# Row numbers of the first expert right after its search, and more of its product in the second search

## The reference

```
logits = x @ w_gate                      # 3072 tokens, 8 experts, 384 columns
take the pairs (token, expert) from the largest logit down; a token goes to
the first expert that still has fewer than 384 tokens
out[mask_e] = max(x[mask_e] @ w1[e], 0) @ w2[e]
```

## Time and profile before

| what | us |
|---|---|
| median of 3 runs (794.68 to 795.75) | 794.81 |
| the profiled execution, its own time | 795.84 |
| its span, first to last instruction | 794.1 |
| TensorE busy in the span | 764.5 |
| VectorE busy in the span | 631.3 |
| mean granted TensorE clock | 0.984 |

### The profile page before, as it was taken

One profiled execution on the slowest core, in us unless ns is written; L12 is line 12 of the kernel. 1 busy time (PEld: TensorE's weight loads), 2 busy tenths in 40 slices (PEclk: granted clock), 3 DMA queues, 4 the chain that ended last, 5 costly groups with the idle time before them and its releaser, 6 DMA issues.

```text
span 794.1 us, 17262 instructions
## 1 busy us (share of the span) xinstructions
PE 764.5 (96%) x6864; PEld 573.2 (72%) x6864; DVE 631.3 (80%) x1081; ACT 425.1 (54%) x703; POOL 292.2 (37%) x244
## 2 busy tenths in 40 slices
PE   8899899999999999999999999977999999999994
PEld 8799678787878787878787877645566565666662
DVE  8998999989998999998999985876776776766220
ACT  2497849595968595968596879410121221222221
POOL 4335462626272627272726260011221231222311
PEclk9999999999999999999999999995999999999998
DMA  9951257373646463656464347123423424415500
GB/s 309 387 201 52 90 203 276 124 270 128 236 164 247 138 235 141 233 192 211 155 220 152 133 154 248 44 73 138 179 98 134 190 66 184 190 46 203 219 31 31
DMA packets 47792, 133.50 MB, mean 168 GB/s; under 512 B 5344, under 2 KB 19808, under 8 KB 45664
## 3 DMA queue, kind: packets, MB, share of 16 engines
q1 hardware_dynamic: 38880, 93.07, 33.4%
q0 software_dynamic: 5376, 34.61, 11.7%
q10 hardware_dynamic: 3456, 4.72, 1.7%
HBM read 97.78 MB, written 34.60 MB: 167 GB/s over the span
## 4 chain that ended last, share of the span: by engine, by line
PE 74%; DVE 10%; issue 2%; ACT 1%; another core or an unknown queue 0%; POOL 0%; ACTq 0%; DVEq 0%
PE bank L425 71%; DVE cmp L1415 2%; PE bank L749 1%; DVE g_lo L1515 1%; DVE t_sb L1118 1%; PE bank L450 1%; PE bank L511 1%; ACT t_sb L826 1%; DVE t_sb L1494 1%; DVE inv L1037 0%; DVE t_sb L1487 0%; DVE t_sb L1490 0%; DVE cum L1028 0%; DVE thr L1432 0%
## 5 line engine op out<-in xcount | busy, mean ns | idle before, releaser
L425 PE MATMUL bank<-x_hi,win_hi 128*128 128x256 f16 (+1 forms) x606 | 159.9, 267 | 0.7 <-DVE x_lo L1100 0.7
L425 PE MATMUL bank<-x_hi,win_lo 128*128 128x256 f16 (+1 forms) x606 | 159.9, 267 | 0.0
L425 PE MATMUL bank<-x_lo,win_hi 128*128 128x256 f16 (+1 forms) x606 | 159.9, 267 | 0.0
L1646 POOL TENSOR_TENSOR g_lo<-t_sb,g_hi 128x512 f16<-128x512 f32 x88 | 123.3, 1428 | 54.3 <-ACT g_hi L826 45.8
L425 PE MATMUL bank<-wout_hi,g_hi 128*128 128x392 f16 (+1 forms) x416 | 129.0, 317 | 1.6 <-DVE wout_lo L1208 1.6
L425 PE MATMUL bank<-wout_lo,g_hi 128*128 128x392 f16 (+1 forms) x416 | 128.8, 316 | 0.0
L425 PE MATMUL bank<-wout_hi,g_lo 128*128 128x392 f16 (+1 forms) x416 | 128.7, 316 | 0.0
L826 ACT ACTIVATE g_lo<-bank 128x384 f16<-128x384 f32 x64 | 31.4, 490 | 143.6 <-PE bank L425 129.1
L1629 POOL TENSOR_TENSOR dv<-v_tok,dot 128x384 f32<-128x384 f32 x24 | 29.0, 1210 | 174.4 <-DVE dot L1067 174.4
L826 ACT ACTIVATE g_hi<-t_sb 128x512 f16<-128x512 f32 x96 | 57.3, 624 | 57.8 <-PE bank L425 53.2
L1118 DVE TENSOR_TENSOR t_sb<-t_sb,h_sb 128x512 f32<-128x512 f32 x96 | 86.5, 947 | 0.5
(11 more groups left out here) (184 smaller groups left out, 1598.2 us busy)
## 6 DMA issues: line engine op xcount, KB each, us to landing
stage<-in_moe_w SPq DMA_DIRECT2D x22, 768.0 KB, 6.4
w_split<-stage SPq DMA_DIRECT2D x22, 768.0 KB, 4.5
fold_w<-in_moe_w SPq DMA_DIRECT2D x10, 768.0 KB, 9.2
w_split<-fold_w SPq DMA_DIRECT2D x10, 768.0 KB, 7.9
wt<-in_w_turned SPq DMA_DIRECT2D x24, 258.0 KB, 2.9
kt<-in_k_turned SPq DMA_DIRECT2D x24, 256.0 KB, 2.6
rt<-in_r_turned SPq DMA_DIRECT2D x24, 256.0 KB, 2.7
r_tok<-in_r SPq DMA_DIRECT2D x24, 192.0 KB, 6.0
```

The costliest lines, as they stand in the source:

```text
L425: return nc.tensor.matmul(*a, **k)
L1646: G.tensor_tensor(g_lo[:, j * GW:(j + 1) * GW], t_sb[:, j * GW:(j + 1) * GW], g_hi[:, j * GW:(j + 1) * GW], ALU.subtract).then_inc(s["glo" ...
```

## The change

The row numbers of the first expert are made at the end of the first search and no longer inside the second. On VectorE `digits`, `numbered`, `one_hot_low` and `id_blocks` stand ahead of the pick, and `token_ids` between the pick and the start of the second search; on TensorE I and J stand behind the first ranks, between 16, 6 and 16 idle products (16 of which were there before). X of the first expert moves from behind the fifth maxima of the second search to behind the third. H0 moves from B5 to B3, H1 to A4, Y0 and H2 to B4, and Y1, H3, Y2, H4 and Y3 follow in that search, so that Y1, H4, Y2 and Y3 move there from the third. The idle products of the second search remain in two steps of four. The third search holds the seven units of the first expert that are left, Y4 to Y7 and H5 to H7, in its first four steps; its units for the second expert stay as they were.

```diff
@@ placement
+        SECOND = {("B", 2): ["X"], ("B", 3): ["H0"], ("A", 4): ["H1"], ("B", 4): ["Y0", "H2"], ("B", 5): ["Y1", "H3"],
+                  ("C", 0): ["Y2", "H4", "Y3"]}
+        THIRD = {("A", 0): ["Y4"], ("B", 0): ["H5"], ("A", 1): ["I", "Y5"], ("B", 1): ["J", "H6"], ("A", 2): ["Y6"],
+                 ("B", 2): ["H7"], ("B", 3): ["Y7"], ("B", 4): ["X"], ("B", 5): ["H0", "H1"],
+                 ("C", 0): ["H2", "Y0", "H3"]}
...
-            for u in PLACES[where]:
-                p = r - 1 if u in YOUNG + ("I", "J") else r - 2
+            for u in {1: SECOND, 2: THIRD}.get(r, PLACES).get(where, []):
+                p = r - 1 if r == 1 or u in YOUNG + ("I", "J") else r - 2
@@ TensorE
-                if r == 1:
-                    idle_products(16)
...
-                    if r == 1 and t < 4:
+                    if r == 1 and t < 2:
                         idle_products(6)
...
                 ranks(r)
+                if r == 0:
+                    idle_products(16)
+                    unit(0, "I", 0)
+                    idle_products(6)
+                    unit(0, "J", 0)
+                    idle_products(16)
                 units(r, ("C", 0), unit)
@@ VectorE
-            def low_xg(p):
+            def low_xg(p, ks=range(KT)):
...
+            def first_search():
+
+                for t in range(NSTEP - 1):
+                    filled(0, t)
+                    next_step(0, t)
+                filled(0, NSTEP - 1)
+                choose(0)
+                take_slots(0)
+                digits()
+                numbered()
+                one_hot_low()
+                id_blocks(0)
+                pick_expert(slice(0, NT))
+                one_hot_expert()
+                token_ids(0)
+                leave()
+                start_search()
+
+            def second_search():
+
+                for t in range(3):
+                    filled(1, t)
+                    next_step(1, t)
+                low_xg(0, range(0, 2))
+                filled(1, 3)
+                low_xg(0, range(2, KT))
+                next_step(1, 3)
+                filled(1, 4)
+                low_h(0, 0)
+                next_step(1, 4)
+                low_h(0, 1)
+                filled(1, 5)
+                low_h(0, 2)
+                choose(1)
+                pick_expert(slice(0, NT), lambda: low_h(0, 3))
+                one_hot_expert()
+                take_slots(1)
+                leave()
+                start_search()
+                digits()
+                numbered()
+                low_h(0, 4)
+
+            first_search()
+            second_search()
+            for r in range(2, E - 1):
...
+                f = 4 if r == 2 else 3
```

More of the change, by code:

```diff
@@ L1516, in low_h @@
                                        ALU.max, ALU.subtract).then_inc(s["hlo"], 1)
-            def low_xg(p):
+            def low_xg(p, ks=range(KT)):
                 if not 0 <= p < E:
                     return
-                for k3 in range(KT):
+                for k3 in ks:
                     dve.wait_ge(s["xgThi"], KT * p + k3 + 1)
@@ L1540, in _ @@
                 link(V.tensor_scalar(grid[t][:, :], iota_t[:, :], wid[:, t:t + 1], None, ALU.mult))
-            for r in range(E - 1):
+            def first_search():
[14 more added lines that the diff above has]
+                start_search()
@@ L1543, in _ @@
+            first_search()
+            second_search()
+            for r in range(2, E - 1):
                 new, old = r - 1, r - 2
-                if r >= 1:
-                    one_hot_low()
+                f = 4 if r == 2 else 3
+                one_hot_low()
                 filled(r, 0)
-                low_h(old, 3)
+                if r > 2:
+                    low_h(old, 3)
                 next_step(r, 0)
                 filled(r, 1)
-                if r >= 1:
-                    id_blocks(r - 1)
@@ L1552, in _ @@
-                low_h(old, 4)
+                id_blocks(r - 1)
+                low_h(old, f + 1)
                 next_step(r, 1)
-                if r >= 1:
-                    token_ids(r - 1)
+                token_ids(r - 1)
                 filled(r, 2)
-                low_h(old, 5)
+                low_h(old, f + 2)
                 next_step(r, 2)
                 filled(r, 3)
-                low_h(old, 6)
+                low_h(old, f + 3)
                 next_step(r, 3)
                 filled(r, 4)
-                low_h(old, 7)
+                if r > 2:
+                    low_h(old, 7)
```

## The result

The changed kernel took 800.02 us (median of 7, 799.49 to 802.76), the kernel before beside it 795.75 (median of 7, 794.68 to 796.93): a ratio of 1.006, interval 1.005 to 1.0071, or 4.3 us more. The forecast was 797.4 with a range up to 799.8. The sign was right, the size too small by 2.6, and the time lies 0.2 outside the range.

A forecast was written before the change was run, and what follows sets the result against it. TensorE, busy 764.5 of 794.1 us, bounds the kernel; the second search is a VectorE-TensorE chain. Half clock: third search starts 3.4 late, 0.8 comes back, so 2.6 on the 794.81 median gives 797.4; range 793.6 to 799.8.

The forecast's parts named there:

- The start: Start of the second search: early row numbers put its first counts at 537.8 instead of 534.20, 3.6 us later.
- the stall: Second search, kernel before: a mark at 546.53 with unknown cause loses 1.8 us; left out of the sum, not certainly gone.
- The main case: Half clock in the second search: third search 3.4 late, 0.8 back, 2.6 us more, so 797.4; chance 0.42.
- the third case: Rival: gather from 536.6 holds the first counts' signal until 540.9, 2.3 more; 799.6 at half clock, 797.7 at full; chance 0.15.
- the other rule: Single GpSimd queue: X's rows stand behind the weights, second gather lands near 542.1, holding the first counts' signal 3.5 us.
- The rows of X: Second search: X's gathered rows arrive by 542.4, before X can start at 544.85, so they cost nothing.
- the 2.4 us in hand: Second search: margin between X's rows arriving at 542.4 and X's start at 544.85.
- H0: Second search, behind the fourth counts: one H part at the half clock takes 2.54 us, fifth counts at 551.3.
- The clock in the second search: TensorE's granted clock falls to half from some point behind 538 until about 552.
- The third search: Loses four parts worth 6.4 us but lasts 30.0 through VectorE's chain, so only 0.8 come back.
- The fourth case: Rival: the third search saves all 6.4 us of the moved parts; 791.8, or 789.8 at full clock; chance 0.16.

The follow-up runs named there:

- row numbers alone: Changed kernel with X, H and Y parts back at their old places and idle products in four steps; only the early row numbers remain: 796.4 us, ratio 1.0028.
- X without the gathers: Changed kernel with the first expert's rows fetched by SyncE from fixed rows, not GpSimd; 799.13 us (ratio 1.0066), then 801.06 and 800.75 in one execution each.
- more idle products: Changed kernel with 28 idle products behind J instead of 16, and 13 instead of 6 in the second search's first two steps: 798.65 us, ratio 1.0046.
- four parts alone: Kernel before, with late row numbers and late X, but Y1, H4, Y2 and Y3 moved behind the second search's ranks: 800.62 us, ratio 1.0061.
- changed order with its clock kept: Changed kernel with idle products added in gaps of the second and third search and 28 instead of 16 behind J: 797.13 us, ratio 1.0035.

## Why the prediction was wrong in size and right in sign

The first counts of each step, forecast for the half clock and measured in the first profile of the change:

| first counts of | forecast | measured | late |
|---|---|---|---|
| second search, step 1 | 537.8 | 537.49 | -0.3 |
| step 2 | 540.7 | 541.73 | 1.0 |
| step 3 | 543.5 | 544.57 | 1.1 |
| step 4 | 547.0 | 547.91 | 0.9 |
| step 5 | 551.3 | 552.44 | 1.1 |
| step 6 | 557.0 | 558.20 | 1.2 |
| third search | 566.1 | 566.78 | 0.7 |

**The start, right.** 3.3 late against the kernel before, for 3.6. The row numbers alone show it as well; they get 1.1 back in the first step and cost 2.0.

**The step that failed: the stall was counted as gone.** The main case starts from 562.67, a start of the third search in which the kernel before has its stall of 1.8, and adds to it a chain without any stall. So where it says that the stall "is not in this sum", it credits the change with 1.8. Measured, the stall had moved to the first mark: from first to second counts it took 4.24 us, where the forecast has 2.9 and the row numbers alone, whose mark is on time, take 2.71. That is 1.3 to 1.5 us, the largest single miss in the traces. It was the third case, to which I gave 0.15, and its price was set too high (2.3, or 3.5 by the other rule), since the mark came 3.48 after the first gather's issue and not 4.3. (Its 799.6 should read 799.7 by its own terms.) The forecast without the credit is 2.6 + 1.8 = 4.4 more. With no stall on either side the measured difference is 4.7 (X without the gathers, first run); with one on both sides it is 4.3 and 3.7 (the two measurements of the change).

**The rows of X, right in cost.** X did not wait in the profile. Windows of the changed kernel while weights and rows arrive:

```profile
538.00:541.00 3.00, 1.22 (x16) 0.88 (x13) 0.86 (x4) 0.00 (x0) 1.48 (x2) 0.87 0.98 418
541.00:543.00 2.00, 1.48 (x29) 0.90 (x28) 1.20 (x4) 0.00 (x0) 0.00 (x0) 0.50 0.80 300
543.00:545.80 2.80, 2.33 (x32) 1.50 (x31) 1.90 (x6) 0.00 (x0) 0.00 (x0) 0.50 0.02 7
```

The DMA share is 0.98 up to 541, 0.80 up to 543 and 0.02 behind that. But the 2.4 us in hand were too many: with more idle products X began at 544.39 after a wait of 0.21 for its rows, so they were there near 544.3 and not 542.4. The Trainium skill, DMA: Bandwidth & Descriptors, section SWDGE vs HWDGE vs iDMA, says that the GpSimd path has one queue. The shares fit rows that stand behind the weights, but rows mixed with the weights would end as late; no run tells the two apart. The mark at 539.80 didn't wait for the rows, so the 3.5 drawn from that rule was no price of this hold.

**H0, mis-sized.** 5.07 for H0 and H1 was halved to 2.54 for one at the half clock. That row straddles the rise of the clock at 557.3. One part wholly at the half clock takes 3.04, which is 0.5 more; its step grew by 0.2 only.

**The clock in the second search, right.** Half from 540.2 to 553.9, forecast from behind 538 to 552. That the third search then starts only 0.7 late is in part luck: behind the sixth counts it took 8.58 us for 9.1, which covers a third of the held mark.

**The third search, right where the clock stays up.** 30.34 for 30.0, the steps 4.99, 5.14, 4.97 and 3.18 for 4.6, 5.1, 4.9 and 3.2, then 4.49 and 7.57 for 4.6 and 7.6. The four parts alone confirm it. But the sum prices every part of this search at the full clock, while the same paragraph puts waits of 0.6 to 0.95 us ahead of Y4, Y5 and Y6. The clock that decided the second search was never asked about the third. It fell there in nine of the eleven profiles that have the early numbers and the moved parts, in six of them for 3.4 us, which costs 1.7, and in three for 6.8. (The four parts alone have the same third search with the late numbers, and the one profile of it has no fall.) This is a second term at nothing without a reason; in the median it is worth at most 0.6.

**The sum.** 797.4 was reckoned from 794.81. Of the 2.6 that lacked, 0.9 are the base (794.81 was the median of three, that of seven is 795.75). 1.0 is the difference of the two profiles, 3.65 for 2.6: 0.7 at the start of the third search, where the held mark is the largest part, and 0.3 in it. The last 0.6 is the difference of the medians, 4.3, less that of the profiles, 3.65, and by the mean clocks it goes with the second fall. A case of its own for that fall would have stood at 799.1, with a range of 798.2 to 800.1.

**Why it is slower at all.** With idle products in both kernels the order costs 4.5 by the medians, and near 3.8 by the executions at the same mean clock. The kernel before pays 1.7 for its clock, the changed kernel 1.3 to 2.0 for its own (ratio 1.0051 to 1.006 against 1.0035), so by the medians the difference at the clocks that they get is again 4 to 5. By the two profiles the order's price is the late start (533.85 to 537.38, 3.5) and 1.3 for a second search of 26.09 instead of 24.80, in which most of the four added parts did fall into gaps, less 0.7 for a third search that takes 30.5 without its fall instead of 31.19. That is 4.1. These profiles are of two chips, C and D, so the parts of the sum are good to a few tenths. The fourth case (four parts saved in full) is out: it needed a third search near 25.

## What to carry to other kernels

Parts that are moved out of a stage shorten it only down to the chain of the other engine, so work out the chain of the stage that loses them before counting them as a gain; here 6.3 went in and 1.5 came out. When a stall in the kernel before has no known cause, it is part of the time that you count from: leaving it out of the new sum counts it as saved, so give the case in which it stays, at full price, a chance of its own. Gaps that an edit opens in a stage at the full clock can let the clock fall there, and a profile in which it doesn't fall is one execution: put the fall into the range with its price. And before a reordering is tried to fill idle time at a low clock, try idle products: they made the kernel before 0.2% faster, and no order tried for the same gaps has a median below that, with the same idle products added or without.

## What the runs showed of the hardware

- The granted clock can fall in a stage that had it in full before an edit opened gaps of 0.3 to 1 us in it, and it does so in some executions and not in others: the third search of one and the same kernel took 30.34 in one profile and 32.01 in the next. That the gaps are the cause was not shown by itself: the runs with idle products in most of them still fell, behind the two gaps of 0.7 that were left.
- A part of nine products of 384 columns takes 1.62 to 1.64 at the full clock and 3.04 at the half; X takes 1.20 and 2.18. Counts take 0.76 and 0.80, and one bare step 2.83 (changed order with its clock kept) and 2.84 (the change): the narrow products and the chain through VectorE hardly feel the clock.
- A mark on VectorE can start 1.2 to 2.0 us later than its counts explain, while GpSimd issues its gathers (0.8 to 0.9 in later searches): in all four profiles of one chip, and in none of the twelve of three others. The kernel before takes 1.4 to 1.7 more where its profiles show it.
